# Theta's transfer moved forward, its low part split in three on GpSimd, and two DVE steps reordered, in a three-layer kernel on one core

## The reference, cut to what matters

```python
for t in range(S):
    state = alpha[:, :, t, :, None] * state + einsum('bhd,bhe->bhde', k[:, :, t], v[:, :, t])
    y[:, :, t] = einsum('bhd,bhde->bhe', q[:, :, t], state)
...
theta = x @ w_theta
zr, zi = x * cos(theta), x * sin(theta)
y = einsum('ts,bsd->btd', w_tok_r, zr) + einsum('ts,bsd->btd', w_tok_i, zi)
u = x + y
x = u + maximum(u @ w_ch, 0)
...
h = maximum(x @ w_in, 0); u, v = h[..., :512], h[..., 512:]
v_s = einsum('ts,bsd->btd', w_spatial, normalised(v)) + b_spatial
out = (u * v_s) @ w_out
```

## Time and profile before

| | |
|---|---|
| median of 3 runs | 598.52 us |
| lowest, highest | 597.65, 598.63 us |
| profiled execution | 597.77 us, its span 596.0 us |
| busy | PE 582.2, DVE 369.4, ACT 237.1, POOL 199.4 us |
| granted TensorE clock | 1.00 of full speed |

### The profile page before, as it was taken

The page is one execution under the profiler, slowest core; times in us unless marked ns, Lnnn a source line. Parts: engine busy times, 40 slices in busy tenths (PEclk is TensorE's granted clock), DMA queues, the critical chain, the costliest instruction groups (busy, mean ns, idle before and its releaser), DMA issues.

```text
span 596.0 us, 11233 instructions
## 1 busy us (share of the span) xinstructions
PE 582.2 (98%) x4631; PEld 554.5 (93%) x4631; DVE 369.4 (62%) x561; ACT 237.1 (40%) x451; POOL 199.4 (33%) x175
## 2 busy tenths in 40 slices
PE   6899899999999999999999999999999999999998
PEld 5788899999999999999999989999999999989997
DVE  7988996877877877778733466747044714371232
ACT  3767555444544534544443228223222313231110
POOL 2565444232432422422321144536023702361130
PEclk9999999999999999999999999999999999999999
DMA  8943212222321420413032280201020010002002
GB/s 303 339 155 123 79 67 68 92 84 67 107 67 68 142 99 29 145 67 108 1 136 89 86 313 0 80 0 54 27 80 1 27 53 1 1 0 81 1 0 81
DMA packets 20403, 49.54 MB, mean 83 GB/s; under 512 B 1664, under 2 KB 15232, under 8 KB 19840
## 3 DMA queue, kind: packets, MB, share of 16 engines
q1 hardware_dynamic: 20352, 48.81, 23.5%
HBM read 39.37 MB, written 9.44 MB: 82 GB/s over the span
## 4 chain that ended last, share of the span: by engine, by line
PE 89%; DVE 5%; ACT 2%; issue 2%; POOL 1%; DMA 0%; DVEq 0%; ACTq 0%
PE psY L471 21%; PE psC L503 6%; PE psY L610 6%; PE psC L430 5%; PE psS L610 4%; PE psF L610 4%; PE psY L587 4%; PE psS L379 3%; PE psY L597 3%; PE psF L413 3%; PE psF L577 3%; PE psY L577 2%; PE psS L587 2%; PE psC L610 2%; PE psS L597 2%; PE psF L597 2%
## 5 line engine op out<-in xcount | busy, mean ns | idle before, releaser
L1133 POOL TENSOR_TENSOR z_lo<-cos_sin,z_hi 128x768 fp32r<-128x768 f32 x23 | 43.7, 1900 | 104.8 <-ACT z_hi L717 104.8
L1199 POOL TENSOR_TENSOR gated_lo<-u_gated,gated_hi 128x384 fp32r<-128x384 f32 x32 | 32.4, 1012 | 123.7 <-ACT gated_hi L837 123.6
L837 ACT ACTIVATE gated_hi<-u_gated 128x384 fp32r<-128x384 f32 x32 | 16.8, 525 | 79.3 <-DVE u_gated L1068 79.3
L1120 POOL TENSOR_TENSOR akq<-akq 128x512 f32<-128x512 f32 x23 | 27.4, 1192 | 58.3 <-DVE akq L896 58.3
L471 PE MATMUL psY<-tok_r_hi,z_hi 128*128 128x384 f32 x126 | 45.5, 361 | 1.1 <-POOL z_lo L1133 1.1
L471 PE MATMUL psY<-tok_r_hi,z_lo 128*128 128x384 f32 x126 | 42.2, 335 | 0.0
L471 PE MATMUL psY<-tok_i_hi,z_lo 128*128 128x384 f32 x126 | 42.2, 335 | 0.0
L471 PE MATMUL psY<-tok_i_hi,z_hi 128*128 128x384 f32 x126 | 42.2, 335 | 0.0
L471 PE MATMUL psY<-tok_i_lo,z_hi 128*128 128x384 f32 x126 | 42.2, 335 | 0.0
L471 PE MATMUL psY<-tok_r_lo,z_hi 128*128 128x384 f32 x126 | 42.1, 334 | 0.0
L885 DVE TENSOR_TENSOR akq<-akq,after 128x512 f32<-128x512 f32 x24 | 41.5, 1731 | 0.9
(11 more groups left out here) (239 smaller groups left out, 1768.3 us busy)
## 6 DMA issues: line engine op xcount, KB each, us to landing
akq<-akq SPq DMA_DIRECT2D x22, 770.0 KB, 4.4
v<-v_in SPq DMA_DIRECT2D x24, 192.0 KB, 4.5
x_dram<-u_f SPq DMA_DIRECT2D x8, 576.0 KB, 3.7
x_raw<-x_dram SPq DMA_DIRECT2D x4, 1152.0 KB, 5.3
out<-ot SPq DMA_DIRECT2D x24, 192.0 KB, 1.9
raw_tok_r<-w_tok_rT SPq DMA_DIRECT2D x6, 384.0 KB, 7.2
raw_tok_i<-w_tok_iT SPq DMA_DIRECT2D x6, 384.0 KB, 8.7
raw_sp<-w_spT SPq DMA_DIRECT2D x1, 2304.0 KB, 9.2
```

Of the source, the lines that this page charges most:

```text
L1133: pool.tensor_tensor(Z[c][1][:], trigs[g % 2][:], f(Z[c][0][:]), ALU.subtract).then_inc(z_lo, 1)
L1199: pool.tensor_tensor(GA[1][:, j, half(h)], ug[h][:, j], f(GA[0][:, j, half(h)]), ALU.subtract).then_inc(g_lo, 1)
```

## The change

Four edits. Theta's transfer is issued between the decays and the keys and queries of chunk 1. ACT makes theta's high part in three pieces instead of one. POOL makes the low part in three pieces, ahead of the queries of chunk 1, and DVE makes it no longer; PE waits for piece j ahead of the matmuls of tile j. On DVE, the first mask goes ahead of the scaling of keys 1, and the scaling of keys 2 goes ahead of the second mask.

```diff
@@ SP, load_akq
                 if g == 1:
                     sp.dma_start(ALPHA[1], akq[0, 1, :, 0:SCAN]).then_inc(alpha_in[1], 16)
+                    sp.dma_start(raw_theta[:], w_theta.rearrange("(c p) n -> p c n", p=P)).then_inc(theta_in, 16)
                     sp.dma_start(AKQ[1][:, SCAN:], akq[0, 1, :, SCAN:]).then_inc(akq_in[1], 16)
                     return
@@ SP
             load_v(0)
-            sp.dma_start(raw_theta[:], w_theta.rearrange("(c p) n -> p c n", p=P)).then_inc(theta_in, 16)
             load_akq(2)
@@ PE, angles
                 for j in range(CT):
+                    if g == 0:
+                        pe.wait_ge(theta_lo, j + 1)
@@ PE, first chunks
-                if c == 1:
-                    pe.wait_ge(theta_lo, 1)
@@ ACT
                     act.wait_ge(theta_in, 16)
-                    act.activation(WT[0][:], raw_theta[:], ACT.Copy).then_inc(theta_hi, 1)
+                    for j in range(CT):
+                        act.activation(WT[0][:, j], raw_theta[:, j], ACT.Copy).then_inc(theta_hi, 1)
@@ DVE
-            decay_keys(1)
+            decays_back(1)
             dve.wait_ge(const_made, 4)
             mask_scores(0)
+            scale_keys(1)
             decay_queries(1)
             update_state(0)
-            dve.wait_ge(theta_hi, 1)
-            dve.tensor_tensor(WT[1][:], raw_theta[:], f(WT[0][:]), ALU.subtract).then_inc(theta_lo, 1)
             decays_back(2)
             xT_low(0)
+            scale_keys(2)
             mask_scores(1)
-            scale_keys(2)
             decay_queries(2)
@@ POOL
+            for j in range(CT):
+                pool.wait_ge(theta_hi, j + 1)
+                pool.tensor_tensor(WT[1][:, j], raw_theta[:, j], f(WT[0][:, j]), ALU.subtract).then_inc(theta_lo, 1)
             scale_queries(1)
             tok_low(0)
```

## The result

| | before | after |
|---|---|---|
| median, first measurement (6 executions each) | 598.48 us | 600.08 us |
| ratio, 95% interval | | 1.0023 [1.0012, 1.0034] |
| median, second measurement on another occasion (27 and 5 executions) | 598.13 us | 600.34 us |
| ratio, 95% interval | | 1.0040 [1.0026, 1.0053] |
| profiled execution, its span | 597.77, 596.0 | 598.86, 597.0 us |

The change makes the kernel slower. The medians differ by 1.60 us where 0.85 was forecast, and the first interval lies on both sides of the 0.2% that was called the limit of what can be told, the second beyond it. The lowest executions differ by 0.99, the profiled ones by 1.09. The ratios are estimates over the executions and not quotients of the medians. One of the six executions of the kernel before took 953.26 us; without it the median is 598.44.

The account below looks back on a forecast made before the run. TensorE's unbroken run, begun at 35.84 us behind mostly VectorE pieces, was taken to bound the kernel; POOL waits and the swap, less the 1.21 saved, gave +0.85: 598.62 profiled, 599.4 us on the median, range 597.5 to 600.2.

Parts of the forecast that it names:

- rival B: Theta's transfer lands late, from 8.35 us on, so POOL's pieces hold DVE longer: +1.2, 599.7 us; chance 0.17.
- Transfers: Theta lands between 7.35 and 8.3 us, keys and queries by 9.55, V at 10.0; costs 0.
- ACT: The 1.16 us copy becomes three pieces of about 0.5, done by 9.4 us in ACT's idle time; costs nothing.
- DVE and POOL: Three POOL pieces and keys 2 ahead of the mask make DVE's second scan of chunk 2 end at 20.35, not 19.50.
- the pattern of the prediction itself: DVE instructions reading two SBUF tensors and POOL's take turns: whichever asked first goes first, the other waits until it finishes.
- The waiting term: DVE's waits for POOL, less the removed subtraction's own 1.21 us, up to the second scan of chunk 2: +0.85 us.
- Keys 1: DVE's scaling of keys 1, issued at 10.2, waits for POOL's piece two, ends at 11.25, recorded with some 1.0 us.
- The mask: DVE's first mask runs from 9.05 to 10.27 us, since PE's 1.16 us of score products are ready by then.
- PE: Scores 1 start at 14.5, not 13.60; angles come 0.2 us early, worth nothing because DVE ends last.
- The shift carries one for one: A shift near 19.4 us, where DVE begins to reduce chunk 0's angle, reaches the kernel's end in full.
- Rival A: DVE gets past POOL in time, xT's low part ends before 15.4, angles come 0.52 us earlier: 598.0 us; chance 0.22.
- Rival C: The plain reading: the DVE subtraction's own 1.21 us goes and nothing is paid: 597.3 us; chance 0.04.

Follow-up runs that it names:

- keys 2 last: Changed kernel with the scaling of keys 2 put back behind the second mask on DVE; median 598.86 us, ratio to before 1.0011.
- PE was started early: Changed kernel with POOL filling the zero tile first and PE multiplying it with itself five times ahead of the transposes; median 599.13 us, ratio to before 1.0019.
- early transfer and mask only: Changed kernel with theta's low part back on DVE, ACT's copy in one piece, keys 2 behind the second mask; median 600.97 us, ratio to before 1.0030.
- the kernel with writes: Changed kernel with POOL's three subtractions replaced by three writes of zero to the same pieces; median 598.4 us, ratio to before 1.0003.

## Why the prediction was right, and where it was short

The time of the first measurement lies in the range (597.5 to 600.2), and slower was forecast, by 0.85 us. That of the second, 600.34, lies 0.14 above it. The mechanism holds in the profiled execution; that the first median falls inside is in part luck, since its 1.60 us are beyond the forecast's 1.1 and rival B's 1.2, and only the 0.5 added for the spread takes it in. Step by step:

- *Transfers.* Theta was to land between 7.35 and 8.3, taken as 8.0; it is issued at 2.18 and lands 5.8 later, at 8.0. Keys and queries land at 2.66 + 6.6 = 9.3, ahead of 9.55. V landed at 3.19 + 6.6 = 9.8 and held nothing up. One rate was misread: the fastest part before was V, 192 KB in 0.45 us, or 427 KB per us and not 372; theta's lower bound would be about 7.15, and nothing hangs on it.
- *ACT.* Three pieces in 1.35 us from 8.02, hidden, as forecast.
- *DVE and POOL.* Forecast and measured: keys 1 end at 11.25 and 11.26; piece three at 12.05 and 12.12; the second scan at 13.2 and 13.21; the scan of chunk 2 at 15.57 and 15.55; xT's low part at 16.0 and 16.00; keys 2 at 17.82 and 17.71; the second scan of chunk 2 at 20.35 and 20.26. The last difference is a wait of POOL that was left out: its token weights were taken to end 1.84 after their issue at 15.43, but by the pattern of the prediction itself they wait for the scan of chunk 2 and end 1.62 after 15.57, at 17.19; the earlier trace rows show it already, with 2.11 us for the 1.84. Measured is 17.16, 1.61 after the scan. The waiting term, forecast +0.85, measures +0.76; with keys 2 last it is -0.27, so 1.03 of it is the swap of keys 2 and the mask. The scan for which no row existed does wait: by the rule cited from the Trainium skill ("SBUF — State Buffer", "Who interferes with whom"), the trace after agrees, with 1.82 us for the scan where it is 1.29 alone.
- *Keys 1.* Expected with some 1.0 us, recorded with 0.70. The mask was 0.37 late, so most of the wait passed before they were issued. Same end.
- *The mask.* "So they are ready by then", of PE's first scores, failed. They took 1.44 us instead of 1.16, the mask started at 9.42, and in other executions at 10.05 to 10.2. I had taken from one profile that PE's products have one duration, while the new order puts one of them on DVE's path. In this execution it cost nothing, since POOL's piece was the later wait.
- *PE.* This is the step that failed: "the 0.2 is worth nothing: DVE ends last". PE's wait for the scores grew from 0.32 to 1.29 us, which I had in the sum (14.5 instead of 13.60) but priced only as a delay. Behind it the granted clock fell to half from 15.3 to 18.7, the angles ended 1.1 late and ACT, not DVE, was last: +0.23 more, and with the 0.08 by which neighbours on DVE overlapped before, 1.07. That the longer wait made the clock fall is not shown: with keys 2 last PE waited 1.68 us and the clock didn't fall there.
- *The shift carries one for one.* Right for the profiled execution: 1.07 at 20.49, 1.07 at 36.91, 1.0 in the span, 1.09 in the time. The distance from there to the end is 560.0 to 560.2 in nine of the profiles; the others have a later fall of the clock (561.5 to 561.7) or, in one case, an earlier one (559.6).
- *From the profiled execution to the median.* I moved the sum by the 0.75 between the two and held the rest equal. But the changed kernel has the fallen clock in 10 of 11 executions and the kernel before in 15 of 91 on three later occasions. A fall near 15 us cost 0.23 in the changed kernel's first profile, nothing when PE was started early, and 1.3 (the time for which DVE waited for ACT) in the kernel with early transfer and mask only; one at 71 us cost 1.4 to 1.6. DVE's waiting for POOL shifts the second scan of chunk 2 by 0.76 us in the first profile of the changed kernel and by 0.34 in the second. So how the 1.60 us of the medians divides between waiting and clock is not settled: only two executions of the changed kernel were profiled, one with a fall at 15 and one with a fall at 71.

The chances were less good than the range: slower by over 0.2% had 0.15, and the two measurements, 1.0023 and 1.0040, say that it was at least as likely as not.

Rival A did not happen; the kernel with writes showed that it does once the second scan isn't held. Rival B did not happen: theta was in time. Rival C, the plain reading, was wrong by 2.3 us in the profiled execution.

## What to carry to other kernels

Before an instruction is moved to GpSimd, list the two-input VectorE instructions that run beside it: each of them that is issued behind it waits for what is left of it, and the longer durations of the same instruction elsewhere in the trace give the price. Swapping two instructions of one engine is not free when one of them can run beside another engine's work and the other can't; here that swap alone made DVE 1.1 us late. And where an edit lengthens a wait of TensorE, look at what the clock does behind it, over several executions, and not only at the wait; the length of the wait alone didn't tell it here.

## What the runs showed of the hardware that was not expected

- Two idle stretches of PE close together, of 0.59 and 1.29 us within 2.5, were followed by half the clock from 15.3 to 18.7 us; in the kernel before, 0.58, 0.32 and then 1.15 (ahead of 16.50) in the same place were not. But the length of the idle time doesn't decide it: with keys 2 last, 0.59 and 1.68 were followed by no fall there, and after 0.59 and about 0.77 the clock fell in the kernel with early transfer and mask only and not in the one with writes. The pair of 0.85 and 1.05 us near 70 was followed by a fall in four of the profiled executions and by none in others with the same idle times, among them the kernel before. What decides between them was not found.
- The products for the first scores, behind the same work of PE, took 1.16 to 1.20 us in some of the profiled executions, 1.44 and 1.57 in two and 2.08 in four. With PE started 2.4 us earlier they took 1.16 in all three kernels profiled that way, and the kernel before was not faster for it.
- POOL's first token weights, a two-input instruction too, ended 1.61 to 1.64 us after DVE's scan of chunk 2 in nine profiles, though they had been issued anything from 0.24 to 0.85 us ahead of the end of that scan. Where DVE holds it, an earlier issue on POOL gains nothing.
- Three writes of 128x384 on POOL (1.24 us) were over at 10.12, before keys 1 and the second scan began (0.68 and 1.29 us). What a write does to a two-input instruction beside it was not seen.
